# The start of a fused attention mix and two MLPs: first mixing on one engine, second softmax on another

## The reference

```
w = exp(weight_gen - max over taps); w = w / (sum over taps + 1e-9)    # (2, 4096, 8 heads, 7 taps)
x1[s, h, :] = sum over k of w[s, h, k] * x[s - 6 + k, h, :]            # zeros ahead of each batch; 24 features a head
x2 = leaky_relu(x1 @ w_in, 0.01) @ w_out                               # 8192 x 192 -> 2048 -> 192
out = elu(x2 @ w2_in) @ w2_out                                         # 192 -> 2048 -> 192
```

## Time and profile before

| | us |
|---|---|
| median of 3 runs | 1156.99 |
| the profiled execution | 1156.67 |
| its span, first to last instruction | 1154.9 |
| PE busy | 1133.8 (98%) |
| VectorE busy | 673.9 (58%) |
| ScalarE busy | 750.0 (65%) |
| GpSimd busy | 422.4 (37%) |

### The profile page before, as it was taken

The page is one execution under the profiler, slowest core; times in us unless marked ns, Lnnn a source line. Parts: engine busy times, 40 slices in busy tenths (PEclk is TensorE's granted clock), DMA queues, the critical chain, the costliest instruction groups (busy, mean ns, idle before and its releaser), DMA issues.

```text
span 1154.9 us, 22749 instructions
## 1 busy us (share of the span) xinstructions
PE 1133.8 (98%) x9804; PEld 920.9 (80%) x9804; DVE 673.9 (58%) x690; ACT 750.0 (65%) x846; POOL 422.4 (37%) x409
## 2 busy tenths in 40 slices
PE   7999999999999999999999999999999999999998
PEld 4878887888878888887888878888887888888886
DVE  7766647456474655647456474564646556464554
ACT  4667758566575765757667575665657667575764
POOL 5745723608044080632707135090541806200000
PEclk9999999999999999999999999999999999999999
DMA  6313021120112102021020111101121020010000
GB/s 176 123 45 94 15 66 29 34 75 29 53 29 80 29 28 67 16 79 28 28 80 28 54 29 53 56 28 53 28 80 29 28 68 27 28 28 28 15 28 28
DMA packets 44723, 55.45 MB, mean 48 GB/s; under 512 B 4116, under 2 KB 32914, under 8 KB 44624
## 3 DMA queue, kind: packets, MB, share of 16 engines
q1 hardware_dynamic: 44624, 54.01, 15.3%
HBM read 36.29 MB, written 17.69 MB: 47 GB/s over the span
## 4 chain that ended last, share of the span: by engine, by line
PE 89%; DVE 4%; ACT 4%; issue 1%; POOL 1%; DMA 0%; SPq 0%; POOLq 0%; ACTq 0%
PE y_a_rows L614 28%; PE hidden L546 28%; PE y_b L607 19%; PE hidden L550 9%; PE hidden L575 5%; DVE hid_lo L1132 2%; DVE act L1107 2%; ACT hid_hi L920 1%; ACT act L904 1%; DMA xw<-in_x_dram 0%; ACT ya L878 0%; DVE up_b_lo L1020 0%; POOL prod L338 0%; POOL act L341 0%; POOL staged L338 0%
## 5 line engine op out<-in xcount | busy, mean ns | idle before, releaser
L614 PE MATMUL y_a_rows<-hid_hi,dn 64*128 64x512 f32 x2048 | 564.3, 386 | 0.0
L607 PE MATMUL y_b<-hid_hi,dn 64*128 64x512 f32 x1024 | 395.9, 387 | 0.5 <-PE y_b L607 0.2
L607 PE MATMUL y_b<-hid_lo,dn 64*128 64x512 f32 x1024 | 395.4, 386 | 0.0
L614 PEld LDWEIGHTS y_a_rows<-hid_hi,dn 64*128 64x128 f32 x2048 | 330.6, 184 | 39.7
L614 PE MATMUL y_a_rows<-hid_lo,dn 64*128 64x512 f32 x1024 | 353.5, 386 | 0.0
L1132 DVE TENSOR_TENSOR hid_lo<-hidden,hid_hi 128x1024 fp32r<-128x1024 f32 x128 | 156.5, 1223 | 206.6 <-ACT hid_hi L920 206.5
L1132 DVE TENSOR_TENSOR hid_lo<-act,hid_hi 128x1024 fp32r<-128x1024 f32 x127 | 172.1, 1355 | 169.7 <-ACT hid_hi L920 169.4
L902 ACT ACTIVATE hidden<-hidden 128x1024 f32<-128x1024 f32 x127 | 128.2, 1009 | 173.0 <-PE hidden L550 173.0
L314 POOL TENSOR_TENSOR mix<-xw,wk 128x384 f32<-128x384 f32 x30 | 38.8, 1294 | 549.3 <-DVE wk L1048 543.9
L904 ACT ACTIVATE act<-hidden 128x1024 f32<-128x1024 f32 x127 | 130.4, 1026 | 132.2 <-PE hidden L550 124.5
L546 PE MATMUL hidden<-in_a_hi,up_a_hi 64*128 64x512 f32 x1020 | 202.8, 394 | 8.8 <-DVE act L1107 5.6
(11 more groups left out here) (108 smaller groups left out, 1195.4 us busy)
## 6 DMA issues: line engine op xcount, KB each, us to landing
xw<-in_x_dram SPq DMA_DIRECT2D x14, 960.0 KB
raw_b<-squares_out SPq DMA_DIRECT2D x60, 96.0 KB, 2.2
out_dram<-staged SPq DMA_DIRECT2D x15, 384.0 KB, 2.6
squares_in<-prod SPq DMA_DIRECT2D x56, 96.0 KB, 2.0
squares_out<-ya SPq DMA_DIRECT2D x15, 256.0 KB, 2.1
raw_a<-squares_in SPq DMA_DIRECT2D x14, 256.0 KB, 2.7
raw_d<-in_moe_w_out_dram SPq DMA_DIRECT2D x8, 384.0 KB, 3.4
raw_a<-in_moe_w_in_dram SPq DMA_DIRECT2D x8, 256.0 KB, 3.6
```

What stands on the lines that cost most here:

```text
L607: return nc.tensor.matmul(y_b[:, :], dn[m][rows, f, P:2 * P], v[rows, s % HB, HALF[i]], start=start, stop=stop)
L614: return nc.tensor.matmul(bank[:, :], dn[m][rows, f, first:first + P], v[rows, s % HB, HALF[i]], start=(f == 0 and n == 0), stop=(f == FT ...
```

## The change

VectorE mixes all four tokens of chunk 0, from tap 6 (the token itself) down to tap 0. The parts of taps 6 to 3 that need no padding rows come before the wait for the padding; 13 instructions in place of 10. GpSimd's share of it goes. In softmax 1 VectorE keeps the max and the reciprocal; the difference, the sum over taps as four sums and one sum with the small constant, and the last product go to GpSimd (`softmax_one`, seven instructions), ahead of its raising of `s_mix`. `wk1` is loaded after the rows of x have arrived. ScalarE rounds in_b of chunk 0 first and copies in_b_up from it, and PE waits for that copy by itself. In the steps of `ASIDE`, 0 and 9, the leaky function writes to `act` in SBUF, and PE waits for it, not for the residual, ahead of steps 2 and 11.

```diff
+        top = ya[0][:, 0:J * H * 3].rearrange("p (a k) -> p a k", k=3)
...
-        FIRST_TERMS = ((prod, 1), (prod2, 2), (mix, 5), (term4, 10))
+        FIRST_TERMS = ((prod, 1), (prod2, 5), (mix, 8), (term4, 13))
-        J_POOL = 1
...
+        ASIDE = (0, ST + 1)
...
-        def first_mixing(eng, ops, j0, j1, done):
...
                 sp.dma_start(xw[lo + 1:hi, 0:PAD, :], x_rows[lo:hi - 1, (ROWS - PAD) * D:]
                              .rearrange("p (j d) -> p j d", d=D)).then_inc(s_x, 16)
+            sp.wait_ge(s_x0, 16)
             load_w(1)
-            sp.wait_ge(s_x0, 16)
             sp.wait_ge(s_x, x_arrived(0))
             load_up(0, 0)
             load_up(0, 1)
...
+            def softmax_one():
+                w, total = wk[1], top[:, :, 0]
+                pool.wait_ge(s_max1, 1)
+                nc.gpsimd.tensor_tensor(w[:, :, :], w[:, :, :], wmax[:, :].unsqueeze(2).broadcast_to((P, J * H, TAPS)), ALU.subtract).then_inc(s_soft1, 1)
+                pool.wait_ge(s_exp, 2)
+                nc.gpsimd.tensor_tensor(top[:, :, :], w[:, :, 0:3], w[:, :, 3:6], ALU.add).then_inc(s_soft1, 1)
+                pool.wait_ge(s_soft1, 2)
+                nc.gpsimd.tensor_tensor(total, top[:, :, 0], top[:, :, 1], ALU.add).then_inc(s_soft1, 1)
+                pool.wait_ge(s_soft1, 3)
+                nc.gpsimd.tensor_tensor(total, total, top[:, :, 2], ALU.add).then_inc(s_soft1, 1)
+                pool.wait_ge(s_soft1, 4)
+                nc.gpsimd.tensor_tensor(total, total, w[:, :, 6], ALU.add).then_inc(s_soft1, 1)
+                pool.wait_ge(s_soft1, 5)
+                nc.gpsimd.tensor_scalar(wsum[:, :], total, EPS, None, ALU.add).then_inc(s_soft1, 1)
+                pool.wait_ge(s_rec1, 1)
+                nc.gpsimd.tensor_tensor(w[:, :, :], w[:, :, :], wrec[:, :].unsqueeze(2).broadcast_to((P, J * H, TAPS)), ALU.mult).then_inc(s_soft1, 1)
-                pool.wait_ge(s_soft, SOFT_STEPS * (c + 1))
+                if c == 1:
+                    pool.wait_ge(s_soft1, 7)
+                else:
+                    pool.wait_ge(s_soft, SOFT_STEPS * (c - 1))
...
                 nc.gpsimd.sem_inc(s_mix, 1)
-            pool.wait_ge(s_x0, 16)
-            pool.wait_ge(s_x, x_arrived(0))
-            pool.wait_ge(s_soft, SOFT_STEPS)
-            first_mixing(pool, nc.gpsimd, J - J_POOL, J, s_term)
-            pool.wait_ge(s_term, FIRST_STEPS)
+            softmax_one()
+
             pool.wait_ge(s_termv, FIRST_STEPS)
             nc.gpsimd.sem_inc(s_mix, 1)
             nc.gpsimd.memset(xw[:, 0:PAD - J, :], 0.0).then_inc(s_pad, 1)
...
                 product(1, up_b_hi, in_b, start=False, stop=False)
+                pe.wait_ge(s_xup, 1)
                 low, high = up_pair(0, input_of(0, 0), 0, stop=True)
                 low.then_inc(s_up1, 1)
...
-                    pe.wait_ge(s_term, steps)
...
-                    if of_two == 0:
+                    if g - 2 in ASIDE:
+                        pe.wait_ge(s_leak, ST * c_two + (s - 2) % ST + 1)
+                        if g == 2:
+                            pe.wait_ge(s_leak1, 1)
+                    elif of_two == 0:
...
+                elif c == 0:
+                    nc.scalar.activation(in_b[n][0:D2, :], b, ACT.Copy).then_inc(s_xhi, 1)
+                    act_e.wait_ge(s_xhi, 2)
+                    nc.scalar.activation(in_b_up[n][D2:P, :], in_b[n][0:D2, :].bitcast(f32), ACT.Copy).then_inc(s_xup, 1)
...
-                    nc.scalar.activation(hidden[:, s % 2, :], hidden[:, s % 2, :], ACT.Prelu, alpha=SLOPE).then_inc(s_leak, 1)
+                    if g in ASIDE and g >= 2:
+                        act_e.wait_ge(s_lo, g - 1)
+                    nc.scalar.activation((act if g in ASIDE else hidden)[:, s % 2, :], hidden[:, s % 2, :], ACT.Prelu, alpha=SLOPE).then_inc(s_leak, 1)
...
-                nc.scalar.activation(hid_hi[:, s % HB, :], (act if m else hidden)[:, s % 2, :], ACT.Copy).then_inc(s_hi, 1)
+                nc.scalar.activation(hid_hi[:, s % HB, :], (act if m or g in ASIDE else hidden)[:, s % 2, :], ACT.Copy).then_inc(s_hi, 1)
-                    nc.scalar.activation(hidden[:, 0, HALF[i]], hidden[:, 0, HALF[i]], ACT.Prelu, alpha=SLOPE).then_inc(signal(s_leak, s_leak1, i), 1)
+                    nc.scalar.activation(act[:, 0, HALF[i]], hidden[:, 0, HALF[i]], ACT.Prelu, alpha=SLOPE).then_inc(signal(s_leak, s_leak1, i), 1)
...
-            def mixing_share():
+            def first_mixing():
+                def product(k, dst, j0, j1):
+                    src = xw[:, k + j0:k + j1, :].rearrange("p j (h g) -> p (j h) g", h=H)
+                    w = wk[0][:, j0 * H:j1 * H, k:k + 1].broadcast_to((P, (j1 - j0) * H, GROUP))
+                    nc.vector.tensor_tensor(dst[:, j0:j1, :].rearrange("p j (h g) -> p (j h) g", h=H), src, w, ALU.mult).then_inc(s_termv, 1)
+                def add(dst, term):
+                    nc.vector.tensor_tensor(dst[:, :, :], dst[:, :, :], term[:, :, :], ALU.add).then_inc(s_termv, 1)
                 dve.wait_ge(s_x0, 16)
+                dve.wait_ge(s_soft0, SOFT_STEPS)
+                product(6, prod, 0, J)
+                product(5, prod2, 1, J)
+                product(4, mix, 2, J)
+                product(3, staged_rows, 3, J)
                 dve.wait_ge(s_x, x_arrived(0))
-                dve.wait_ge(s_soft, SOFT_STEPS)
-                first_mixing(dve, nc.vector, 0, J - J_POOL, s_termv)
+                product(5, prod2, 0, 1)
+                product(4, mix, 0, 2)
+                product(3, staged_rows, 0, 3)
+                dve.wait_ge(s_termv, 7)
+                add(mix, staged_rows)
+                product(2, term4, 0, J)
+                product(1, term5, 0, J)
+                dve.wait_ge(s_termv, 8)
+                product(0, staged_rows, 0, J)
+                dve.wait_ge(s_termv, 10)
+                add(term4, term5)
+                dve.wait_ge(s_termv, 12)
+                add(term4, staged_rows)
...
+                nc.vector.tensor_tensor(hid_lo[:, s % HB, :], (act if m or g in ASIDE else hidden)[:, s % 2, :], hid_hi[:, s % HB, :].bitcast(f32), ALU.subtract).then_inc(s_lo, 1)
...
-            mixing_share()
+            first_mixing()
             split_up(0, 0)
+            dve.wait_ge(s_w[1], 16)
+            nc.vector.reduce_max(wmax[:, :], wk[1][:, :, :], AX_X).then_inc(s_max1, 1)
+            mlp1_input_lo(0, 0)
             split_up(0, 1, (0,))
-            mlp1_input_lo(0, 0)
-            softmax_a(1)
             mlp1_input_lo(0, 1)
-            softmax_b(1)
             split_up(0, 1, (1,))
+            dve.wait_ge(s_soft1, 6)
+            nc.vector.reciprocal(wrec[:, :], wsum[:, :]).then_inc(s_rec1, 1)
```

More of the change, by code:

```diff
@@ L152, in attention_leaky_elu_mlps @@
         s_id = sem("identity_ready")
+        s_soft0 = sem("first_softmax_steps")
+        s_soft1 = sem("second_softmax_steps_gpsimd")
+        s_max1 = sem("second_softmax_max")
+        s_rec1 = sem("second_softmax_reciprocal")
         s_soft = sem("softmax_steps")
@@ L155, in attention_leaky_elu_mlps @@
         s_mul = sem("mix_steps")
-        s_term = sem("first_mix_steps_gpsimd")
         s_termv = sem("first_mix_steps_vector")
@@ L161, in attention_leaky_elu_mlps @@
         s_xhi = sem("mlp1_input_hi")
+        s_xup = sem("first_input_b_high_rows")
         s_xin = sem("mlp1_input_ready")
@@ L820, in softmax_exp @@
             def softmax_exp(c):
-                act_e.wait_ge(s_soft, SOFT_STEPS * c + 2)
+                if c == 0:
+                    act_e.wait_ge(s_soft0, 2)
+                elif c == 1:
+                    act_e.wait_ge(s_soft1, 1)
+                else:
+                    act_e.wait_ge(s_soft, SOFT_STEPS * (c - 2) + 2)
                 nc.scalar.activation(wk[c % 2][:, :, :], wk[c % 2][:, :, :], ACT.Exp).then_inc(s_exp, 1)
@@ L1031, in softmax_a @@
             def softmax_a(c):
                 dve.wait_ge(s_w[c % 2], 16 * (c // 2 + 1))
-                done = SOFT_STEPS * c
-                nc.vector.reduce_max(wmax[:, :], wk[c % 2][:, :, :], AX_X).then_inc(s_soft, 1)
-                dve.wait_ge(s_soft, done + 1)
+                steps, done = (s_soft, SOFT_STEPS * (c - 2)) if c else (s_soft0, 0)
+                nc.vector.reduce_max(wmax[:, :], wk[c % 2][:, :, :], AX_X).then_inc(steps, 1)
+                dve.wait_ge(steps, done + 1)
                 nc.vector.tensor_tensor(wk[c % 2][:, :, :], wk[c % 2][:, :, :], wmax[:, :].unsqueeze(2).broadcast_to((P, J * H, TAPS)),
-                                        ALU.subtract).then_inc(s_soft, 1)
+                                        ALU.subtract).then_inc(steps, 1)
@@ L1039, in softmax_b @@
             def softmax_b(c):
-                done = SOFT_STEPS * c
+                steps, done = (s_soft, SOFT_STEPS * (c - 2)) if c else (s_soft0, 0)
                 dve.wait_ge(s_exp, c + 1)
-                nc.vector.reduce_sum(wsum[:, :], wk[c % 2][:, :, :], AX_X).then_inc(s_soft, 1)
-                dve.wait_ge(s_soft, done + 3)
```

(14 more changed lines are left out.)

## The result

The changed kernel takes 1161.03 us, the median of 6 runs (1159.22 to 1163.95), beside 1156.99 (1156.29 to 1157.21) for the kernel before in 6 runs: ratio 1.0037 with a 95% interval of 1.0024 to 1.005: slower by 0.37%. The prediction was 1159.5, its range 1157.2 to 1163.4. The profiled execution took 1161.25 us with a span of 1159.1, before 1156.67 and 1154.9.

The account below looks back on a forecast made before the run. PE bounds the body, so only the start and step 9's stall count: 1.8 (late quarter 2) + 1.4 (clock) - 0.65 (step 9) = +2.55 us, predicted 1159.5 us, range 1157.2 to 1163.4.

Parts of the forecast that it names:

- Mixing: Start, VectorE: first mixing runs from 5.54 to 14.8 us, ending 3.4 us earlier, a lead that does not reach the path.
- In_b first: ScalarE's copies at the start: rounding in_b ahead of in_b_up gains nothing (between 0 and 0.6 us).
- Small steps: Second softmax on GpSimd: five small steps at 0.28 us each, 1.4 in all (0.7 to 4.9), ending at 20.1.
- rival C: Small softmax steps on GpSimd cost 0.98 us each, ending 3.5 later: 1163.0 us; counts from 0.4 a step; chance 0.16.
- The signal: GpSimd's first-chunk signal, behind the second softmax, leaves at 21.1 us; SP issues chunk 1's rows 2.9 later (2.6 to 6.6).
- The clock: PE step 3, after 8 us idle: 3.4 us at half pace makes step 4 1.4 us later (0 to 3.1).
- Second limit: Mixing(1) on GpSimd waits for chunk 1's rows, ends at 54.9; PE, turning at 56.0, finds it done.
- Rival B: No clock loss after PE's idle gap; mixing(1) then holds PE: 1158.5 us, down to 1158.1; chance 0.27.
- Step 9: PE ahead of step 11 waits for the leaky step, not the residual of step 9: gains 0.65 us, not 1.0.
- the quarter's delay: Up-weight quarter 2 lands 2.9 us later behind the late signal; ScalarE waits; step 4 comes 1.8 us later.
- rival D: Faster: the 3.4 us lead reaches step 4, plus 0.65 from step 9: 1152.9 us; chance 0.06.

Follow-up runs that it names:

- VectorE's queue cleared: Mixing on VectorE alone plus step 9 aside, with in_b rounded first, its residual right behind in_a's, down weights rounded before the exponential: 1153.79 us.
- the run with PE kept busy: The changed kernel with 32 added matmuls of 512 columns, output unread, on PE ahead of step 3: 1159.31 us.
- The best kernel: The kernel before with only the first mixing on VectorE alone, the later load of wk1 and step 9 aside: 1153.25 us, ratio 0.997.

## Why the prediction was right, and where its terms were off

The mechanism held: a signal that came too late, a ScalarE that waited for a transfer, a PE that idled and then ran at half clock. Its terms:

- **Mixing**: 5.6 to 14.8 us forecast, 5.57 to 14.82 measured. As the prediction said, its lead didn't reach the path; alone, with the signal early, it is worth 2.65 us.
- **In_b first**: nothing forecast (0 to 0.6). In the changed kernel it can't show, since everything waits for quarter 2. With VectorE's queue cleared one trace has 0.56 at the turning, and the medians show nothing.
- **Small steps**: 0.28 us each forecast; three of 32 columns lasted 0.24 to 0.31 and the TENSOR_SCALAR 0.31, but the first (96 columns) 0.56, and each start follows the last one by 0.32 to 0.64 us. They took 0.41 each with their waits, just where rival C was to begin to count, and ended at 20.86, not 20.1. The prediction's estimate of some 0.2 us for 32 columns, from the Trainium skill (GPSIMD Engine Reference, section 3.1), comes out low against the 0.24 to 0.31 of the trace; the page has a figure for the dispatch on VectorE alone. The estimate's 1.1 us for the five also took the first for 32 columns, and it has 96. Rival C, at 0.98 each, did not come.
- **The signal**: 21.1 forecast, 21.33 measured, by two errors that cancel: the steps were 0.8 late, but the signal leaves as the last product starts, not as it ends. The near hit is luck. The zeroing of the padding does wait for the product's end (21.85), and SP waits for it before the padding rows and so before quarter 2: 3.46 later than before, not 2.9. That is 0.56 of the error, and step 3 is 0.6 later than forecast (33.10 for 32.5).
- **The clock**: the low stretch was set at 3.4 us, the length that followed a gap of 2.34 us. After 8.13 us of idle it lasted some 10 us, mostly under the idle PE; 4.4 us of it, from 33.1 to 37.5, fell on step 3. Against before, step 3 is 2.45 later and step 4 is 4.20 later: 1.75 for the clock, net of the 0.3 of waiting that it covers, for 1.4 forecast.
- **Second limit**: not binding, as forecast (done at 53.82, PE there at 56.91), and shown to be there when the first is taken away.
- **Rival B** (no loss of clock) is out by the granted clock and by the run with PE kept busy.
- **Step 9**: 0.65 forecast, 0.5 measured (PE 4.06 us late ahead of it, 3.58 behind, and the same in the two other pairs of runs).

So +2.55 was forecast, and the trace shows +3.58 at step 11: 0.65 from quarter 2, 0.35 from the clock, 0.17 from step 9, less 0.14 that the steps from step 4 to step 9 give back. From there to the last down products the shift grows from 3.58 to 3.98, which is not of the change: between the same two instructions of VectorE, at 108.5 and 947.0 us in the kernel before, the 14 profiled executions of the study last from 838.0 to 839.1 us, whatever their start. At the last instruction the shift is 4.14. The two errors of most size have one direction: the quarter's delay, which the prediction took from the signal alone and not from what SP waits for behind it, and the clock's cost.

One judgement of the prediction was not tested by its outcome: it gave step 0 aside no cost of its own. In the changed kernel, where the residual of step 0 lasts 1.23 us and everything waits for quarter 2, nothing speaks against that, but no run took step 0 aside out of it alone. With that wait gone it costs 2.8 us alone and some 1.5 in the kernel with the signal first (1.9 and 1.2 in the timelines, at the turning). Of its rival D, 1152.9 for a signal ahead of 18.2 us, only 1155.2 was to be had, mostly for this reason: without step 0 aside it is 1153.4.

## What to carry to other kernels

A signal that lets another queue load goes ahead of any work that waits for something, and so does whatever else that queue waits for; here one call moved behind the signal and the zeroing was worth 6.1 us. A buffer that is freed early is not free of cost: look at which memories the consumer's operands then lie in, and at whether two short gaps of PE join into one long one. A cause removed tells nothing of the change's other parts: each was worth its own run, and the sum of the good ones was found that way.

## What the runs showed that I had not expected

**A residual is dearer with both inputs in SBUF.** The page after groups both kinds of residual: the mean of those that read `act` (SBUF) is 1358 ns, of those that read `hidden` (PSUM) 1223; the page of before has the same difference, 1355 ns, and I passed over it.
```profile
L1172 DVE TENSOR_TENSOR hid_lo<-hidden,hid_hi 128x1024 fp32r<-128x1024 f32 x126 | 154.1, 1223 | 212.1 <-ACT hid_hi L932 212.0
L1172 DVE TENSOR_TENSOR hid_lo<-act,hid_hi 128x1024 fp32r<-128x1024 f32 x129 | 175.2, 1358 | 172.4 <-ACT hid_hi L932 172.1
```
The residual of step 0 lasted 1.23 us in the changed kernel, where GpSimd stood waiting, and 1.53, 1.66, 1.71, 1.82 and 1.90 where it was mixing; GpSimd's own sum beside the 1.90 took 1.99 instead of 1.0. The Trainium skill (SBUF — State Buffer, "SBUF: two separate sides") says that a VectorE instruction with two SBUF inputs and a GpSimd one that reads SBUF exclude each other, and that whoever comes second waits for the whole of the other; the trace agrees that both lose, with 0.3 to 0.7 us on VectorE and 1.0 on GpSimd.

**The run's time goes with its mean granted clock, loosely.** In the changed kernel the span was 1157.4 us at a mean clock of 0.996, 1158.3 and 1159.0 at 0.995, 1159.0 and 1159.1 at 0.993, and 1162.0 at 0.992. With step 0 aside it was 1153.2 to 1153.4 at 0.998 and 1155.7 and 1156.1 at 0.994, but at 0.996 anything from 1153.4 to 1155.5. The best kernel, whose profile has no gap of PE over 1.22 us behind the mixing, stayed at 0.998 to 0.999, and its six spans within 0.8 us. But short gaps don't ensure this: the one with the mixing alone has the same gaps in its profile and spans from 1151.4 at 0.999 to 1154.6 at 0.996, and the one with in_b's way cleared one of 1154.7 at 0.998. A part lies at the end of the kernel, which no experiment touched: from the first to the last of its eight last small products' starts it is 2.37 us in the changed kernel, where the clock is 0.50 from 1155 us, and 1.64 in the run with PE kept busy, where it is 0.96 from 1150 to 1155. That and the 1.1 us of the long stretch above are still less than the 2 to 3 us by which single runs are longer; what makes the rest stays open.
